# The end of an empty run in a computed tile order: set to zero where the tile that frees a weight slot is worked out

## The reference

```
def _moe2_ref(x, w_gate, w1, w2):        # x 1536x512, w1 8x512x1024, w2 8x1024x512
    logits = x @ w_gate
    expert_idx = np.argmax(logits, axis=1)
    ...
    for e in range(E):
        mask = expert_idx == e
        if not mask.any():
            continue
        xe = x[mask]
        h = np.maximum(xe @ w1[e], 0.0)
        ye = h @ w2[e]
        out[mask] = gate_w[mask, None] * ye
```

## Time and profile before

| what | value |
|---|---|
| time, median of 3 runs | 917.83 us (917.58 to 917.97) |
| the profiled execution's own time | 919.6 us |
| its span in the trace | 917.6 us |
| PE busy | 806.7 us, 88% |
| DVE, ACT, POOL busy | 61%, 53%, 49% |
| last stage, 19 tile steps | from 589.5 us to the end |

### The profile page before, as it was taken

How to read it: one execution, slowest core, us unless ns; L and a number is a source line. 1 busy time by engine, 2 the same in 40 slices (tenths; PEclk the granted TensorE clock), 3 DMA queues, 4 the chain that set the end, 5 groups by cost and what they waited for, 6 DMA issues and landing times.

```text
span 917.6 us, 13297 instructions
## 1 busy us (share of the span) xinstructions
PE 806.7 (88%) x4246; PEld 708.7 (77%) x4246; DVE 564.2 (61%) x962; ACT 489.3 (53%) x971; POOL 454.2 (49%) x402
## 2 busy tenths in 40 slices
PE   3699999999998899999999999598888868898885
PEld 2588989898978789999999889486666656776664
DVE  2478888888976787888887887452432323423322
ACT  2378877887897887886877784300113121111100
POOL 2222456345465874774764542743546384333380
PEclk9699999999999999999999999598989889989989
DMA  8598887886626609319501307440506054224020
GB/s 170 124 221 190 186 176 174 190 187 141 187 61 204 216 21 344 109 53 339 185 1 49 135 1 252 156 156 24 207 12 217 18 191 143 88 70 159 1 76 17
DMA packets 72387, 125.01 MB, mean 136 GB/s; under 512 B 33438, under 2 KB 36094, under 8 KB 68224
## 3 DMA queue, kind: packets, MB, share of 16 engines
q1 hardware_dynamic: 64816, 92.28, 37.9%
q10 hardware_dynamic: 5024, 25.56, 8.0%
q0 software_dynamic: 2480, 6.31, 1.8%
HBM read 60.26 MB, written 34.24 MB: 103 GB/s over the span
## 4 chain that ended last, share of the span: by engine, by line
PE 71%; POOL 9%; ACT 7%; issue 4%; DVE 3%; DMA 2%; ACTq 2%; SPq 1%; POOLq 0%
POOL split L763 7%; PE ps L1326 6%; PE ps L1415 5%; PE ps L1416 5%; PE ps L1414 4%; PE ps L1400 4%; PE ps L1399 4%; PE ps L1398 4%; PE ps L1560 3%; PE ps L1316 3%; PE ps L1317 3%; PE ps L1338 3%; ACT split L909 3%; PE ps L1339 3%; PE ps L1561 3%
## 5 line engine op out<-in xcount | busy, mean ns | idle before, releaser
L763 POOL TENSOR_TENSOR split<-wraw,split 128x512 f32 (+1 forms) x112 | 139.2, 1279 | 151.7 <-ACT split L909 148.2
L909 ACT ACTIVATE split<-wraw 128x512 f32 (+1 forms) x128 | 68.9, 618 | 237.7 <-PE ps L1586 125.9
L1057 DVE TENSOR_TENSOR ptl<-ps,pth 128x512 fp32r<-128x512 f32 x144 | 98.8, 686 | 35.5 <-ACT pth L847 33.6
L740 POOL TENSOR_TENSOR hw<-hw,ha 128x384 f32<-128x384 f32 x64 | 65.3, 1020 | 76.8 <-ACT hw L921 76.8
L847 ACT ACTIVATE pth<-ps 128x512 fp32r<-128x512 f32 x144 | 86.7, 602 | 30.9 <-PE ps L1326 30.8
L1037 DVE TENSOR_REDUCE negmax<-ps 128x1 f32<-128x768 f32 x96 | 91.1, 949 | 15.1 <-PE ps L1317 15.1
L1560 PE MATMUL ps<-split,xth 128*128 (+1 forms) x152 | 68.1, 448 | 27.7 <-POOL split L763 25.4
L1584 PE MATMUL ps<-split,hth 128*128 (+1 forms) x152 | 65.5, 431 | 29.3 <-POOL split L763 26.5
L1326 PE MATMUL ps<-cst,pr 128*128 128x128 f32 x576 | 88.2, 273 | 1.0 <-ACT pr L838 1.0
L1398 PE MATMUL ps<-xh,wih 128*128 128x384 f32 x256 | 86.9, 339 | 2.0 <-DVE hp L1091 2.0
L838 ACT ACTIVATE pr<-ps,negmax 128x768 f32<-128x768 f32 x96 | 86.8, 904 | 3.2 <-DVE negmax L1037 3.2
(11 more groups left out here) (195 smaller groups left out, 2060.9 us busy)
## 6 DMA issues: line engine op xcount, KB each, us to landing
routed<-blank SPq DMA_DIRECT2D x33, 771.0 KB, 14.9
wraw<-in_moe_w ACTq DMA_DIRECT2D x24, 1024.0 KB, 5.8
wraw<-in_moe_w SPq DMA_DIRECT2D x8, 1024.0 KB, 5.4
operand<-qk_hi SPq DMA_DIRECT2D x16, 384.0 KB, 4.8
operand<-qk_lo SPq DMA_DIRECT2D x32, 192.0 KB, 4.3
operand<-qk_hi SPq DMA_DIRECT2D x32, 192.0 KB, 4.5
operand<-mask SPq DMA_DIRECT2D x16, 384.0 KB, 5.1
xg<-routed SPq DMA_DIRECT2D x19, 256.0 KB
```

What stands on the lines that cost most here:

```text
L763: pool.tensor_tensor(split_piece(E_LO[x], ring, k), wraw[:, x, i, :], split_piece(E_HI[x], ring, k).bitcast(F32), ALU.subtract).then_inc(e ...
L909: act.activation(split_piece(E_HI[x], ring, k), wraw[:, x, i, :], ACT.Copy).then_inc(e_hi[x], 1)
L1057: dve.tensor_tensor(ptl[:, at:at + CW], ps[:, 4 + c % 2, :], pth[:, at:at + CW].bitcast(F32), ALU.subtract).then_inc(ptl_done, 1)
```

## The change

The end of each run is multiplied by the flag that says whether the run holds a tile. Where it does, the end is as before; where it doesn't, the end is zero instead of equal to the run's start. One DVE instruction with two inputs becomes one with three; no instruction is added, removed or moved on any engine.

```
-            dve.tensor_tensor(span[on, 1:2], span[on, 0:1], runs[on, 1:2], ALU.add).then_inc(seg_dve, 1)
+            dve.scalar_tensor_tensor(out=span[on, 1:2], in0=span[on, 0:1], scalar=runs[on, 1:2], in1=runs[on, 0:1], op0=ALU.add, op1=ALU.mult).then_inc(seg_dve, 1)
```

## The result

The changed kernel took 839.63 us (median of 4 runs, 838.92 to 840.65) where the kernel before, run beside it, took 917.71 (917.26 to 917.97). The ratio is 0.915, 95% interval 0.914 to 0.917: 78.1 us less. Forecast were 837.6 us, 80.2 less. The profiled execution has a span of 837.1 us and a time of 838.99.

What follows compares the result with a forecast made beforehand. PE's waits for POOL's weight splits were taken to bound the last stage. Removing 51.9 us of waiting and 28.3 of half clock, 80.2 us, from the median 917.83 gave 837.6 us, range 836.3 to 843.0.

Steps and rivals of the forecast that it cites:

- What bounds the stage: Last stage: PE waits 12 times, 51.9 us, for POOL's weight splits, let go only by the other stream's tile.
- The values of the table: Ends of ranks 2 to 7 become 1, 4, 7, 8, 11, 14, 1 or 2 lower; ACT's w1 copies start accordingly.
- the narrow place: Rank 5's w1 in front of mm1 of tile 10: ready 708.4, wanted 710.2, so 1.8 us to spare.
- The loads are what is late: For rank 5's w1, loads set the limit: 12.45 us from POOL's end of the previous w2 to its w1 end.
- the first rival: One stall stays: rank 5's w1 comes too late through its load or the scatter; 839 to 845 us, 8%.
- The step of 12.34 us: PE runs the last stage's tile steps at 12.34 us without pause; 0.3 us a step, 5 us, kept for range.
- The sum: turn_h(2) to turn_h(18): 277.44 us before, 197.26 after, 80.2 less, taken off the median 917.83.
- Behind turn_h(18) nothing changes: The end of the kernel, behind the last tile's turn_h, was to take the same time as before.
- The split into 51.9 us of waiting and 28.3 of half clock: The 80.2 us gain in the last stage as PE's waiting plus slower matmuls behind 12 stalls, 2.4 us each.
- no effect: Rival: something other than the empty runs sets the greatest end, `tab_end` stays, 917.9 us; 4%.
- mutual blocking: Rival: DVE and POOL block each other, 8 splits take about 20 us, time about 863 us; 2%.
- half clock throughout: Rival: PE's clock does not hold without pauses; 16 steps at 0.50 would give 998 us; 1%.

Runs made afterwards that it cites:

- the two delays: Changed kernel with POOL doing rank 5's first w1 piece two times more (843.1 us, one run) or four times more (845.36 us).
- the second comparison: Changed kernel, unchanged, run again beside the kernel before: 840.22 us against 916.91 us, ratio 0.916.
- the early end for w1 alone: Changed kernel with `tab_end` (for w2) taken from the starts again, `tab_half` (for w1) keeping the changed ends: 893.25 us, ratio 0.973.
- the kernel with filled stalls: Kernel before with 16 matmuls of 512 columns into an unread PSUM bank in front of each of the 12 waits: 900.6 us, ratio 0.980.

## Why the prediction was right, and where it was off

- **What bounds the stage**: right. (PE's waits of 2.2 and 0.3 us for DVE at the very start, which the prediction left out with "nothing else holds PE there", lie ahead of turn_h(2) and change nothing.) Moving `tab_end` alone, past the empty runs, gave the whole gain, and ACT's starts after the change stand behind the last tiles of their own stream.
- **The values of the table**: right; the w1 copies of ranks 2 to 7 started at 604.2, 628.1, 665.1, 696.0, 718.6 and 751.5, all 1.1 to 2.5 us ahead of the forecast starts. Ranks 3, 4 and 7 were 1.6 ahead, as turn_h(2) itself was, rank 2 0.9 more and ranks 5 and 6 0.3 and 0.5 less.
- **The instruction at no cost**: the changed instruction took 0.21 us, as forecast; whether its 0.06 us more show in the time is not to be told here.
- **No stall left**: right, with the narrow place where it was put. Room of 1.7 to 1.8 us was forecast, 1.65 is in the trace, and the two delays confirm it from the other side. The chain of 12.45 us held: 694.37 to 706.95 is 12.58, of it 0.1 because POOL's sets took 10.05 us instead of 9.95.
- **"The loads are what is late", the reason given for the narrow place**: this was wrong, though its length, read in one piece, was right. The chain holds no transfer. In the kernel before, the second load of w1 of rank 5 was issued at 695.15 and landed 7.7 us later, at 702.9, while POOL was still at the w2 before until 704.04 and the copy of w1 came at 705.68. In the chain stand the scatter, the issue of a w2 load that waits for POOL, and ACT's first copy. So the first rival, a load that lands later, had almost 3 us more room than was said.
- **The step of 12.34 us**: right, 218 us of it without a pause. The 5 us kept for slower steps were not needed.
- **The sum**: the stage's forecast length of 197.26 us was 196.91; the 0.35 is the last step, 818.32 - 806.51 = 11.81 where 12.16 was forecast. Off was what it was taken from. 277.44 us of before is one execution; another had 275.72 with the same waits. The forecast's 80.2 is 78.8 by that one.
- **"Behind turn_h(18) nothing changes"**: this step failed. The last mm2 ran partly at half clock behind a pause of 2.7 us that had been harmless in both traces of the kernel before, 1.65 us. Six of the nine traces with that pause show the fall. With it the two traces give 80.5 - 1.65 = 78.9 and 78.8 - 1.65 = 77.2; measured were 78.1 and, in the second comparison, 916.91 - 840.22 = 76.7. The other executions have no trace, so how many of them had the fall is not known.
- **Luck**: the profiled span came out at 837.1 us where 837.4 was forecast, but only since turn_h(2) came 1.6 us earlier, which the change has no part in, and hid the 1.65 us of the tail. The median was 2.0 us above the forecast.
- **The split into 51.9 us of waiting and 28.3 of half clock**: too simple, though the sum did not rest on it. Filling the pauses took 277.44 - 259.57 = 17.9 us off the stage (17.3 by the medians), not 28. Three terms make up most of the difference. Each wait delays PE by 0.24 us more than its bracket says (4.36 against 4.12 above), 3 us over twelve, so the half clock was 25 rather than 28. Two waits grew by 1.76 us each when PE came earlier. And behind these two the clock fell again, 20.06 - 12.34 - 6.12 = 1.6 us each.
- **The rivals**: one stall, no effect, mutual blocking and half clock throughout are all ruled out by the rows above; the sets of POOL are 1% longer, not twice as long.

What stays open is why the clock falls behind the last pause in one execution and not in another. It fell in six traces and stayed in three, behind the same 2.70 us. The three had a half-clock stretch behind a stall earlier in the stage, but so had two of the six. That the change brings the fall about is thus not shown, and the early end for w1 alone, with eight stalls left, speaks against it.

## What to carry to other kernels

When a consumer waits for work that is released by a table or a counter, find by the timeline which event lets the producer go, and ask whether that event is needed: here it was a tile of the other stream, and one tile of lead was worth 8.4% of the time. Model the fixed chains (here issue of a load, copy, split) beside the unstalled pace of the consumer and look for the smallest room. Read what stands in such a chain, too: here a copy stood behind the issue of a load that it did not need. The smallest room, and not the share of idle time, tells how many stalls go. A gain of this kind should be summed over whole steps from one joint to the other, and taken from more than one execution, since the cost of the clock behind a pause varies.

## What the runs showed of the hardware

- The same pause of PE of 2.70 us was followed by half clock in the last mm2 in six traces and not in three (tails of 18.8 and 17.1 us). In the kernel with filled stalls, two waits of 2.22 us with 3.90 us of filler ahead of them were followed by it too, ten of 0.7 us were not.
- The cost of the half clock behind the same twelve waits differed by 1.7 us between two executions of the same program (275.72 and 277.44 us). It is not the only thing that varies: turn_h(2), ahead of all stalls, came at 621.41 and 623.49 us in the two traces of the changed kernel.
- POOL's 8 splits took 10.03 to 10.05 us in the stage without stalls and 9.90 to 9.96 in the kernel before; no run shows why. At a place with 1.7 us to spare it counts.
- A load of 1 MB into `wraw` landed 5.5 us after its issue, and the one issued half a microsecond behind it 7.7 us after (rank 5 in the kernel before). In the changed kernel the second took 7.9.
